# Fused clustered attention and two MLPs on one core: first weight loads moved back, centroids loaded ahead of k, and calls around the two changes of stage put in another order

## What is computed

```python
q_assign = argmax(q_n @ c_n.T); k_assign = argmax(k_n @ c_n.T)      # 16 centroids per head
scores = where(q_assign == k_assign, q @ k.T / 8, -1e9)             # batch 2, heads 8, 768 tokens, depth 64
x = softmax(scores) @ v                                             # 16 heads in all -> [1536, 512]
h = x @ w_in                                                        # MLP 1: 512 -> 2048 -> 512
x = where(h >= 1, h, where(h <= -1, 0, (h + 1) ** 2 / 4)) @ w_out
xn = x / sqrt(mean(x * x) + 1e-6) * rms_g                           # MLP 2: 512 -> 1536 -> 512
out = (silu(xn @ w_gate) * (xn @ w_val)) @ w_out2
```

## Time and profile before

| | before |
|---|---|
| median of 3 runs | 818.58 us (816.81, 818.58, 820.59) |
| the profiled execution, its own time | 821.07 us |
| its span in the trace | 819.2 us |
| PE busy | 801.0 us |
| DVE, ACT, POOL busy | 639.1, 490.4, 402.5 us |
| mean granted clock of TensorE | 0.994 |

### The profile page before, as it was taken

One profiled execution on the slowest core, in us unless ns is written; L12 is line 12 of the kernel. 1 busy time (PEld: TensorE's weight loads), 2 busy tenths in 40 slices (PEclk: granted clock), 3 DMA queues, 4 the chain that ended last, 5 costly groups with the idle time before them and its releaser, 6 DMA issues.

```text
span 819.2 us, 15394 instructions
## 1 busy us (share of the span) xinstructions
PE 801.0 (98%) x5369; PEld 736.0 (90%) x5369; DVE 639.1 (78%) x1221; ACT 490.4 (60%) x894; POOL 402.5 (49%) x356
## 2 busy tenths in 40 slices
PE   7899999999999999999999999999999999999998
PEld 6799999999988889999999899898899999999997
DVE  5799999999997776575665678997767787878666
ACT  2888888888988676655555569877332222222221
POOL 1135443246568853652462465975393673919000
PEclk9999999999999989999999999999999999999999
DMA  8844754755641100200200110200220101110102
GB/s 187 194 108 113 168 131 114 160 125 123 140 109 46 37 1 27 78 1 27 70 8 27 34 45 27 65 26 2 65 66 2 52 1 52 39 27 27 48 31 78
DMA packets 65443, 54.83 MB, mean 67 GB/s; under 512 B 30080, under 2 KB 52608, under 8 KB 65376
## 3 DMA queue, kind: packets, MB, share of 16 engines
q1 hardware_dynamic: 64288, 53.33, 25.5%
q10 hardware_dynamic: 1088, 0.62, 0.3%
HBM read 27.30 MB, written 3.15 MB: 37 GB/s over the span
## 4 chain that ended last, share of the span: by engine, by line
PE 88%; DVE 3%; ACT 3%; DMA 2%; issue 2%; POOL 1%; SPq 1%; ACTq 0%; DVEq 0%; POOLq 0%
PE ps L921 34%; PE ps L949 14%; PE ps L961 12%; PE ps L752 8%; PE ps L735 8%; PE ps L702 4%; PE ps L705 4%; PE ps L770 1%; PE ps L793 1%; PE ps L794 1%; DMA k<-stage 1%; PE ps L816 1%; SPq L536 1%; DVE gl L1930 0%; DMA cnat<-in_centroids 0%
## 5 line engine op out<-in xcount | busy, mean ns | idle before, releaser
L921 PE MATMUL ps<-th,wh 128*128 128x256 f32 x840 | 240.9, 287 | 3.5 <-DVE hid L1904 2.7
L921 PE MATMUL ps<-tl,wh 128*128 128x256 f32 x840 | 239.2, 285 | 0.0
L921 PE MATMUL ps<-th,wl 128*128 128x256 f32 x840 | 239.1, 285 | 0.0
L921 PEld LDWEIGHTS ps<-th,wh 128*128 128x128 f32 x840 | 162.3, 193 | 7.6 <-DVE tl L1732 3.2
L921 PEld LDWEIGHTS ps<-tl,wh 128*128 128x128 f32 x840 | 162.4, 193 | 2.0
L921 PEld LDWEIGHTS ps<-th,wl 128*128 128x128 f32 x840 | 162.3, 193 | 0.0
L2419 POOL TENSOR_TENSOR wl<-wraw,wh 128x448 fp32r<-128x448 f32 x80 | 104.9, 1339 | 1.3
L1745 DVE TENSOR_SCALAR_CACHE_REDUCE sf<-ps 128x768 f32<-128x768 f32 x96 | 91.6, 955 | 15.2 <-PE ps L705 11.8
L1754 DVE TENSOR_TENSOR ptl<-ps,pth 128x512 fp32r<-128x512 f32 x144 | 94.7, 683 | 5.1 <-ACT pth L1163 4.9
L1163 ACT ACTIVATE pth<-ps 128x512 fp32r<-128x512 f32 x144 | 82.8, 588 | 24.8 <-PE ps L752 16.0
L2400 POOL TENSOR_TENSOR wraw<-corner,wraw 128x256 f32<-128x256 f32 x20 | 17.4, 869 | 153.9 <-DMA wraw<-in_moe_w_val 86.0
(11 more groups left out here) (149 smaller groups left out, 1778.5 us busy)
## 6 DMA issues: line engine op xcount, KB each, us to landing
q<-atile SPq DMA_DIRECT2D x32, 192.0 KB, 3.4
k<-atile SPq DMA_DIRECT2D x32, 192.0 KB, 3.3
o1raw<-in_moe_w_out SPq DMA_DIRECT2D x8, 512.0 KB, 3.8
nat<-in_q SPq DMA_DIRECT2D x16, 192.0 KB, 4.0
wraw<-in_moe_w_in SPq DMA_DIRECT2D x24, 128.0 KB, 2.6
vnat<-in_v SPq DMA_DIRECT2D x16, 192.0 KB, 3.3
moved<-osb SPq DMA_DIRECT2D x16, 192.0 KB, 4.2
wraw<-in_moe_w_val SPq DMA_DIRECT2D x24, 128.0 KB, 2.6
```

What stands on the lines that cost most here:

```text
L921: last = pe.matmul(dst[:, 0:HC], a[w][:, j, kt, :], b[c][:, j, kt, :], start=(opened and kt == 0 and i == 0), stop=(kt == KH - 1 and i == ...
```

## The change

Three things are changed, and no instruction is added, removed or altered.

1. On SP, `head0.behind()` is called 14 calls later: after `head0.send_masks()` and before `head1.next_qk()`.
2. On ACT's queue, the centroids are loaded ahead of k of head 0.
3. In the two changes of stage, calls on ACT, DVE, POOL and SP stand in another order. PE's order is the same.

```diff
             pre3, pre2, pre1, head0, head1 = (work(*at(n)) for n in range(-3, 2))
-            head0.behind()
             pre3.next_qk()
...
             head0.next_v()
             head0.send_masks()
+            head0.behind()
             head1.next_qk()
...
             load_up(3)
+            load_up(4)
             load_out1(2)
-            load_up(4)
...
         @block.scalar
         def _(act):
+            act.dma_start(cnat[:, :], cent.rearrange("h c d -> (h c) d")).then_inc(centroids_loaded, 16)
             act.dma_start(nat[:, 0, :, D:P], k_v[0]).then_inc(qk_loaded[0], 16)
-            act.dma_start(cnat[:, :], cent.rearrange("h c d -> (h c) d")).then_inc(centroids_loaded, 16)
```

ACT at the first change of stage:

```diff
             bend(0, 0)
             snap(1)
-            head16.spread_out()
+            second_t_hi(5, 1)
+            second_t_hi(6, 1)
             hidden_hi(0, 0)
             bend(0, 1)
+            head16.spread_out()
+            hidden_hi(0, 1)
+            bend(1, 0)
+            t_hi(2, 0, 1)
+            t_hi(2, 1, 1)
             copy_corner(1)
-            hidden_hi(0, 1)
-            second_t_hi(5, 1)
-            second_t_hi(6, 1)
             second_t_hi(7, 1)
-            bend(1, 0)
             second_t_hi(8, 1)
             second_t_hi(9, 1)
-            t_hi(2, 0, 1)
-            hidden_hi(1, 0)
             second_t_hi(10, 1)
             snap(2)
+            hidden_hi(1, 0)
             bend(1, 1)
```

DVE at the first change of stage:

```diff
             inner_second(1)
+            second_half(1)
             hidden_lo(0, 1)
             second_t_lo(4, 1)
-            second_half(1)
+            first_half(1)
             second_t_lo(5, 1)
             second_t_lo(6, 1)
             second_t_lo(7, 1)
+            maximum(1, 0)
             second_t_lo(8, 1)
-            maximum(1, 0)
+            first_sum(2)
             second_t_lo(9, 1)
-            first_half(1)
             second_t_lo(10, 1)
-            first_sum(2)
+            second_sum(2)
             hidden_lo(1, 0)
```

The second change of stage, cut to the places that matter (ACT at steps 23 and 29 to 31, DVE at step 31, POOL at step 24):

```diff
+            bend(23, 0)
+            bend(23, 1)
             squares(1, 2, 1)
-            bend(23, 0)
+            inverse_out(0)
+            hidden_hi(23, 0)
+            snap(24)
+            hidden_hi(23, 1)
             squares(1, 3, 1)
-            bend(23, 1)
-            hidden_hi(23, 0)
-            inverse_out(0)
-            snap(24)
...
+            hidden_hi(30, 0)
+            take_y(29, 1)
+            take_y(29, 0)
+            snap(31)
+            take_y(29, 3)
+            copy_corner(31)
             take_y(29, 2)
-            take_y(29, 1)
-            hidden_hi(30, 0)
-            snap(31)
-            copy_corner(31)
             silu(31)
-            take_y(29, 3)
...
-            hidden_lo(31, 0)
             first_sum(32)
             second_sum(32)
             inner_first(32)
             inner_second(32)
+            hidden_lo(31, 0)
...
             high_up(10)
+            high_out(8)
+            t_sum(4, 0, 1)
+            t_sum(4, 1, 1)
             low_up(10, 0, 1)
+            low_out(8, 0)
             low_up(10, 1, 1)
-            high_out(8)
-            high_out(9)
-            low_out(8, 0)
-            t_sum(4, 0, 1)
+            t_sum(4, 2, 1)
             low_up(10, 2, 1)
             low_up(10, 3, 1)
-            t_sum(4, 1, 1)
+            high_out(9)
```

More of the change, by code:

```diff
@@ L1517, in _ @@
             t_hi(2, 3, 1)
+            hidden_hi(2, 0)
+            take_y(1, 2)
+            snap(3)
+            take_y(1, 3)
             t_hi(2, 4, 1)
-            take_y(1, 2)
-            hidden_hi(2, 0)
-            snap(3)
             bend(2, 1)
-            take_y(1, 3)
+            copy_corner(3)
+            t_hi(2, 5, 1)
             hidden_hi(2, 1)
-            t_hi(2, 5, 1)
+            bend(3, 0)
             t_hi(2, 6, 1)
-            copy_corner(3)
-            bend(3, 0)
             snap(4)
@@ L1531, in _ @@
             bend(3, 1)
+            copy_corner(4)
             hidden_hi(3, 1)
             bend(4, 0)
-            copy_corner(4)
+            hidden_hi(4, 0)
+            snap(5)
             bend(4, 1)
-            hidden_hi(4, 0)
+            take_y(3, 2)
+            hidden_hi(4, 1)
             take_y(3, 3)
-            take_y(3, 2)
-            snap(5)
-            hidden_hi(4, 1)
+            copy_corner(5)
             bend(5, 0)
-            copy_corner(5)
+            bend(5, 1)
+            snap(6)
             hidden_hi(5, 0)
-            snap(6)
-            bend(5, 1)
+            copy_corner(6)
             hidden_hi(5, 1)
             bend(6, 0)
-            copy_corner(6)
             bend(6, 1)
-            take_y(5, 2)
             hidden_hi(6, 0)
@@ L1553, in _ @@
             hidden_hi(6, 1)
+            take_y(5, 2)
             for s in range(7, 19):
@@ L1568, in _ @@
             squares(0, 1, 1)
+            squares(0, 2, 1)
+            snap(21)
             scale_x(0, 0, 1)
-            snap(21)
-            squares(0, 2, 1)
-            scale_x(0, 1, 1)
             hidden_hi(20, 1)
             squares(0, 3, 1)
+            scale_x(0, 1, 1)
             scale_x(0, 2, 1)
@@ L1580, in _ @@
             t_hi(3, 1, 1)
-            t_hi(3, 2, 1)
             bend(21, 1)
@@ L2171, in _ @@
             maximum(5, 0)
+            maximum(5, 1)
             first_sum(6)
@@ L2178, in _ @@
             second_half(6)
+            first_half(6)
             hidden_lo(5, 1)
-            first_half(6)
             take_y(5, 0)
+            maximum(6, 0)
             take_y(5, 1)
-            maximum(6, 0)
             maximum(6, 1)
@@ L2271, in _ @@
             maximum(23, 0)
-            add_squares(1, 2)
+            maximum(23, 1)
+            add_squares(1, 1)
             first_sum(24)
@@ L2275, in _ @@
             second_sum(24)
-            maximum(23, 1)
+            hidden_lo(23, 1)
             inner_first(24)
             inner_second(24)
-            hidden_lo(23, 1)
             second_half(24)
+            scale_gate(24)
             first_half(24)
+            add_squares(1, 2)
             sums_lo(1)
-            scale_gate(24)
             t_lo(4, 0, 1)
             take_y(23, 1)
+            take_y(23, 3)
             take_y(23, 0)
@@ L2289, in _ @@
             second_sum(25)
+            hidden_lo(24, 0)
             take_y(23, 2)
             inner_first(25)
-            hidden_lo(24, 0)
             inner_second(25)
             second_half(25)
+            first_half(25)
             scale_gate(25)
-            take_y(23, 3)
+            product(25)
             t_lo(4, 1, 1)
-            first_half(25)
-            product(25)
             first_sum(26)
@@ L2328, in _ @@
             first_sum(28)
-            hidden_lo(27, 0)
             second_sum(28)
             inner_first(28)
+            inverse(2)
+            hidden_lo(27, 0)
             inner_second(28)
             second_half(28)
+            first_half(28)
             scale_gate(28)
@@ L2709, in _ @@
             t_sum(5, 1, 1)
+            t_sum(5, 2, 1)
+            t_sum(5, 3, 1)
             high_out(11)
-            t_sum(5, 2, 1)
-            high_out(12)
             low_out(11, 0)
-            t_sum(5, 3, 1)
             sum_up(11)
```

243 lines of the change are left out of this document (118 added, 125 removed).

## The result

The changed kernel took **810.47 us** (median of 4 runs, 809.8 to 811.81); the kernel before, measured beside it again, 819.29 us (816.81 to 820.59). The ratio is 0.9898, with a 95% interval of 0.987 to 0.9926. It was measured in two more series, each beside the kernel before: 0.9942 (0.9923 to 0.9961) and 0.9933 (0.9908 to 0.9958). By these ratios the change wins between 4.7 and 8.4 us, and how much depends on more than the order of the calls. Part of it is TensorE's clock: all 4 executions of the first series have a mean granted clock of 0.996 or more, while 9 of the 15 in the other two have 0.991 or 0.992. Over the three series the ten executions at 0.996 or more have a median of 811.6 us and the nine others one of 814.3.

The account below looks back on a forecast made before the run. PE was taken as the bound, busy 801.0 of 819.2 us, so only its idle and low-clock time could be won. Terms 0.7 + 5.2 + 1.4 = 7.3 us, from 818.58 to 811.3 us; range 808.8 to 815.5.

Parts of the forecast that it names:

- the side with 0.79: Whole kernel: chance given to a measured time under 814.5 us, counted as faster; same had 0.17, slower 0.04.
- Start: First microseconds: centroids issued at 0.76 instead of 1.49, the shift alone counted, 0.7 us won, between 0 and 1.6.
- Weights late: SP's queue at the start: six issues and 1 MB moved later, counted as 0; cost up to 5.4 us if they delayed q and k.
- First change: Step 2: `first_half(1)` moved ahead, so PE's 2.74 us wait and the low clock go; 5.2 us won, between 0.3 and 6.0.
- The 0.8 us that were to be left in the block: Step 2's block: small remaining waits for ACT's corner copy, piece 7 and part 3, subtracted from 6.0 us.
- Second change: Change to MLP 2: three waits of PE, at steps 24, 30 and 33, lose their cause; 1.4 us won, between -1 and 1.9.
- the 0.2 set aside for new waits: Change to MLP 2: 0.2 us subtracted for POOL's narrow margin before the weights of pair 10 and similar places.
- The other moves: SP's later weights, POOL from step 8, DVE from step 4: PE had no idle time there, counted as 0.
- nothing at the start: Rival, start: k or the transposes keep the old pace, 0.7 us less won, 812.0 us; chance 0.12.
- Stretched DVE: Rival, first change: four DVE instructions stretched beside POOL, 2.1 us more remain, 813.4 us; chance 0.12.
- The wait moves: Rival, first change: ACT's late corner copy idles PE over 2 us, clock falls, only 0.3 us won there, 816.2 us; chance 0.13.
- Slower: Rival, step 26: POOL's `t_sum(4, 0)` waits up to 8.2 us for ACT ahead of pair 10's weights, 821.9 us; chance 0.05.

Follow-up runs that it names:

- centroids first alone: Kernel before, with only the centroids loaded ahead of k of head 0, the weights staying at the front of SP's queue: 817.46 us, ratio 0.9987.
- one more move: Changed kernel with `hidden_lo(1, 1)` ahead of `second_half(2)` and `t_lo(2, 0)` on DVE, run together with reordering at step 27: 809.67 us, repeated 810.79 us.

## Why the prediction was right, and where it was wrong

The forecast was 811.3 us, the result 810.47, inside the range and on the side with 0.79. By its own steps:

- **Start, 0.7 us (0 to 1.6): too small.** The rule that was weighed there (lighter load, shorter transfer) pointed to the right end, 1.6, but for another reason. The load was worth 0.7 us of this transfer; being issued ahead of k made it 2.2 us shorter, and that was not in the sum, which has only the 0.7 us of earlier issue. The upper end was too low as well, since ACT was taken to be free at 3.92; it began at 3.29, for its issues and table load moved too. L678 came 2.3 us earlier. By the ratio of the start alone the place gives 1.4 us, in the profiled pair 4.1. The pair had the same low clock in its first 40 us (0.96 in both windows), so 4.1 is what the place gives at best, with a short low clock. The three executions of the new start with 13.7 us of it begin step 0 at 257.4 to 258.5, and the four with the old start at 257.0 to 259.1.
- **Weights late, 0: right in its cost, wrong in a reason.** The text has q and k of head 1 come 3.6 us earlier. They are issued at 4.93 against 5.10 before, since SP waits for the loads of head 0 there in both. That the weights delayed them all the same shows in the 2.80 us wait with centroids first alone: their transfers, and not their issues, are what stood in the way.
- **First change, 5.2 us: the mechanism right, the size drawn from one execution.** The wait of 2.74 us is in every trace with the old order; the low clock after it is not. Up 2 to up 3 takes 16.3 us in the profiled execution of before and 13.8 in three kernels with that very order, where the clock stays at 1.00. So the 2.8 us for the clock were a price to be paid sometimes, entered as a sure one. The 0.8 us that were to be left in the block are 0.3. In their place comes the 1.2 us wait on `hidden_lo(1, 1)`, 1.5 us with its consequences, which the text does not have: it followed the moved calls to the block of step 2 and not to the down product behind it. Together 4.0 us in the profiled pair, 1.5 where both had the full clock, 3.0 by the ratio of the part alone.
- **Second change, 1.4 us: right in its three waits, too small.** They are gone, and the trace gives 2.5 in this stretch. The three blocks were sized as 0.2 + 1.0 + 0.4 us and gave 0.43 + 1.28 + 0.37 (step 24's up block 5.55 to 5.12, the down product of step 30 4.03 to 2.75, step 33's up block 5.40 to 5.03). Small losses in the other blocks of steps 25 to 32 add 0.4, and the 0.2 set aside for new waits were not needed. The margin of POOL at step 26 was enough; no wait for the weights of pair 10 appears. But the place is narrow: in two of the eight profiled executions with the new order the gain is lost again.
- **The other moves, 0:** steps 3 to 20 are 0.3 us shorter, in the scatter of the table. Steps 34 to 59 are 0.4 shorter, and 0.36 of it is the up block of step 34 (5.39 to 5.03), so it belongs to the second change.

Two errors of opposite sign met in the sum: the clock was counted once too often at step 2, and too little was given to the start and the second change. Against the single parts' 5.1 us, 7.3 was 2 too many; the first series' 8.4 is on the other side. The forecast lies between the series of the kernel, and its closeness to the first is in good part luck: in that series no execution had a mean clock under 0.996, and the other two gave 4.7 and 5.5 us where 7.3 were forecast.

The rivals: *nothing at the start* fell with L678 at 4.84. *Stretched DVE* did not happen where it was placed, and it is what happens at step 24 of the third series and in the 1.43 us of `hidden_lo(1, 1)`. *The wait moves* is true in part: to the down product of step 1, with 1.2 us and no fall of the clock in any execution seen. *Slower*, by POOL's `t_sum(4, 0)`, was not seen.

## What to carry to other kernels

Where a wait is removed, follow the engine on which the calls were moved one block further than the wait itself: the next wait (1.2 us here) stood right behind it, and one more move took it away. A low clock that stands behind idle time in one trace is a risk with a share, not a term: look at a second execution before it enters a sum at full price. And of small first transfers, the one that the chain needs goes first on its queue; for this transfer that did more than emptying the other queues (1.9 us against 3.4), though the time of the kernel showed a gain clear of noise only with both.

## What the runs showed that was not expected

- The length of a low clock varies with the same code and the same timing ahead of it: 3.4 us in one execution, 13.7 in another, and it can fall while PE is 4.89 of 5 us busy. Idle time of 2.74 us in one place was followed by it in two of five executions profiled with the old order.
- A transfer of 32 KB took 4.06 us behind one of 192 KB on the same queue, 3.38 with 1 MB of other transfers out of the way, and 1.9 as the first of its queue, where it landed 0.5 us after the first of the weights was issued.
- One DVE instruction on 128x512 elements took between 0.7 and 1.84 us, by where it fell against a POOL instruction of 2.0 us.
